# Tile 0 of a fused two-layer kernel: side-by-side remainders, an early gelu table, later weight chunks, and filler matmuls during the convolution

## What is computed

```python
def _attn_ref(x, weight):                      # x (2, 4096, 192), weight (8, 7)
    w = np.exp(weight - np.max(weight, axis=-1, keepdims=True))
    w = w / (np.sum(w, axis=-1, keepdims=True) + 1e-09)
    x_pad = np.concatenate([np.zeros((B, 6, D)), x], axis=1)
    idx = np.arange(S)[:, None] + np.arange(7)[None, :]
    x_unf = x_pad[:, idx, :].reshape(B, S, 7, 8, 24)
    return np.einsum('hk,bskhg->bshg', w, x_unf).reshape(B, S, D)

def _moe_ref(x, w_in, w_out):                  # w_in (192, 2048), w_out (2048, 192)
    h = x @ w_in
    g = h * (1.0 / (1.0 + np.exp(-1.702 * h)))
    return g @ w_out

def _moe2_ref(x, w_in, w_out, a, b):
    h = x @ w_in
    P = a[0] + a[1] * h + a[2] * h**2 + a[3] * h**3
    Q = 1.0 + np.abs(b[0]) * np.abs(h) + np.abs(b[1]) * h**2
    return (P / (Q + 1e-6)) @ w_out

return _moe2_ref(_moe_ref(_attn_ref(x, weight), ...), ...)
```

## Time and profile before

| | us |
|---|---|
| median of 3 runs | 1370.47 |
| lowest and highest | 1369.91, 1372.64 |
| the profiled execution | 1370.77 |
| its span, first to last instruction | 1368.5 |
| PE busy | 1321.6 |
| DVE busy | 1110.2 |
| ACT busy | 966.7 |
| POOL busy | 322.6 |

### The profile page before, as it was taken

The page is one execution under the profiler, slowest core; times in us unless marked ns, Lnnn a source line. Parts: engine busy times, 40 slices in busy tenths (PEclk is TensorE's granted clock), DMA queues, the critical chain, the costliest instruction groups (busy, mean ns, idle before and its releaser), DMA issues. The chain is left out here.

```text
span 1368.5 us, 14943 instructions
## 1 busy us (share of the span) xinstructions
PE 1321.6 (97%) x4800; PEld 698.8 (51%) x4800; DVE 1110.2 (81%) x1223; ACT 966.7 (71%) x1144; POOL 322.6 (24%) x148
## 2 busy tenths in 40 slices
PE   3999999999999999999999999999999999999885
PEld 2445555555555555555555555555555555555431
DVE  4339898888889888888888888888888888877894
ACT  4337777777777777777777777777777777777683
POOL 3202222222222222222222222222222222222222
PEclk9999999999999999999999999999999999999997
DMA  7100000000000000000000000000000000000000
GB/s 198 52 12 0 12 1 24 1 23 1 12 11 0 23 0 23 0 11 11 0 23 0 23 0 11 11 0 23 0 22 3 12 1 0 12 1 12 0 12 11
DMA packets 32884, 20.38 MB, mean 15 GB/s; under 512 B 10321, under 2 KB 30801, under 8 KB 32849
## 3 DMA queue, kind: packets, MB, share of 16 engines
q1 hardware_dynamic: 32372, 19.93, 5.2%
q10 hardware_dynamic: 477, 0.01, 0.0%
HBM read 13.64 MB, written 6.29 MB: 15 GB/s over the span
## 5 line engine op out<-in xcount | busy, mean ns | idle before, releaser
L729 POOL TENSOR_TENSOR work<-work 128x1024 f32<-128x1024 f32 x128 | 303.4, 2370 | 987.8 <-ACT work L470 936.9
L281 PE MATMUL acc_a<-g,down 128*128 128x512 f32 x1024 | 478.5, 608 | 0.0
L281 PEld LDWEIGHTS acc_a<-g,down 128*128 128x128 f32 x1024 | 183.9, 190 | 293.9 <-issue 293.9
L287 PE MATMUL acc_b<-g,down 128*64 128x512 f32 x1024 | 271.6, 607 | 13.9 <-DVE g L630 12.2
L619 DVE TENSOR_TENSOR work<-work,h 128x1024 f32<-128x1024 f32 x128 | 156.4, 1222 | 136.6 <-ACT work L470 135.8
L457 ACT ACTIVATE work<-h,par 128x1024 f32<-128x1024 f32 x128 | 142.7, 1115 | 171.7 <-PE h L275 170.7
L267 PE MATMUL h<-x_a_hi,up_a_hi 128*128 128x512 f32 x512 | 235.0, 459 | 22.3 <-DVE x_b L601 15.5
L497 ACT ACTIVATE work<-work 128x1024 f32<-128x1024 f32 x128 | 135.9, 1062 | 157.3 <-POOL work L729 156.9
L268 PE MATMUL h<-x_a_lo,up_a_hi 128*128 128x512 f32 x512 | 201.8, 394 | 0.0
L269 PE MATMUL h<-x_a_hi,up_a_lo 128*128 128x512 f32 x512 | 201.3, 393 | 0.0
L270 PE MATMUL h<-x_b,up_b_hi 128*128 128x512 f32 x512 | 200.4, 392 | 0.0
(11 more groups left out here) (80 smaller groups left out, 939.2 us busy)
## 6 DMA issues: line engine op xcount, KB each, us to landing
out<-y_out SPq DMA_DIRECT2D x16, 384.0 KB, 2.5
x_in_a<-in_x SPq DMA_DIRECT2D x16, 256.0 KB, 2.8
down<-in_moe_w_out SPq DMA_DIRECT2D x8, 384.0 KB, 6.6
x_in_b<-in_x SPq DMA_DIRECT2D x32, 64.0 KB, 2.5
work<-in_moe_w_in SPq DMA_DIRECT2D x8, 256.0 KB, 4.3
work<-in_moe_w_in SPq DMA_DIRECT2D x16, 128.0 KB, 4.7
wts<-in_weight ACTq DMA_DIRECT2D x2, 0.4 KB
wts<-in_weight SPq DMA_DIRECT2D x2, 1.3 KB
```

The costliest lines, as they stand in the source:

```text
L281: last = mm(l.acc_a[:], l.down[:, f, 0:P], l.g[:, slot, k, :], start=f == 0, stop=f == STEPS - 1)
L287: return mm(acc_b[l.acc_row:l.acc_row + DB, :], l.down[:, f, P:D], l.g[:, slot, k, :], start=f == 0, stop=f == STEPS - 1)
L729: tt(m, sq[(s - LAG_RATIO) % 2], seed, ALU.mult).then_inc(m_ready, 1)
```

## The change

There are four edits, all for the first tile; the loop over the other tiles is as before.

1. In tile 0 (`v1 < DUOS`), `down_b_apart` takes the place of `down_b` for layer 1: unit k = 0 sums on partitions 64 to 127, unit k = 1 on partitions 0 to 63. So each half holds a sum over 8 units, and DVE adds the halves in step n = 8, with a copy and an addition into a new buffer `x2_part`, before it splits.
2. ACT fetches gelu's table in set-up, by a gelu of one column right behind the Sqrt.
3. ACT takes layer 1's weight chunks 2 and 3 behind the gelus of steps 0 and 1 rather than around the split of x. Layer 2's chunks follow in steps 2, 3, 4 and 5.
4. PE runs three fp32 matmuls of 128x512 (the identity with `xt_a`) into `acc_a` once 13 of the convolution's operations are done. Nobody reads their result.

```diff
-S_WEIGHTS2 = (0, 2, 4, 5)
+S_WEIGHTS2 = (2, 3, 4, 5)
+WARM_AFTER = 13
...
+            def down_b_apart(l, d, slot, k):
+
+                row = l.acc_row if k == 0 else DB - l.acc_row
+                return mm(acc_b[row:row + DB, :], l.down[:, 2 * d + k, P:D], l.g[:, slot, k, :],
+                          start=d == 0, stop=d == DUOS - 1)
...
-                        last_b = down_b(L1, e1, (s - LAG_DOWN1) % 2, k)
+                        unit = down_b_apart if isinstance(v1, int) and v1 < DUOS else down_b
+                        last_b = unit(L1, e1, (s - LAG_DOWN1) % 2, k)
...
             pe.wait_ge(x_evacuated, 2)
+            pe.wait_ge(conv_steps, WARM_AFTER)
+            for _ in range(3):
+                mm(L1.acc_a[:], ident[:], xt_a[:, HALO:], start=True, stop=True)
...
             fn(root[:, 1:2], root[:, 0:1], ACT.Sqrt).then_inc(setup_act, 1)
+            act.wait_ge(setup_act, 3)
+            fn(stat[:, 0:1], root[:, 1:2], ACT.Gelu_apprx_sigmoid)
             weights_hi(L1, 1, stage1, w1_hi)
-            weights_hi(L1, 2, stage1, w1_hi)
             split_x1(0, 0)
-            weights_hi(L1, 3, stage1, w1_hi)
...
                     step(i, s, i % 2)
+                    if i == 0 and s < 2:
+                        weights_hi(L1, 2 + s, stage1, w1_hi)
                     if i == 0 and s in S_WEIGHTS2:
                         weights_hi(L2, S_WEIGHTS2.index(s), stage2, w2_hi)
...
                 if s == S_X2 and tile_live(t):
                     dve.wait_ge(acc1_b_done, t + 1)
                     wait(dve, h2_ready, DUOS * (t - 1))
-                    nc.vector.tensor_copy(L2.x_b[DB:P, 1 - p, :], acc_b[DB:P, :]).then_inc(x2_b_hi_done, 1)
+                    whole = acc_b
+                    if isinstance(t, int) and t == 0:
+                        whole = x2_part
+                        nc.vector.tensor_copy(x2_part[DB:P, :], acc_b[0:DB, :]).then_inc(x2_part_read, 1)
+                        dve.wait_ge(x2_part_read, 1)
+                        tt(x2_part[DB:P, :], acc_b[DB:P, :], x2_part[DB:P, :], ALU.add).then_inc(x2_part_added, 1)
+                        dve.wait_ge(x2_part_added, 1)
+                    nc.vector.tensor_copy(L2.x_b[DB:P, 1 - p, :], whole[DB:P, :]).then_inc(x2_b_hi_done, 1)
                     dve.wait_ge(x2_b_hi_done, t + 1)
-                    tt(L2.x_b[0:DB, 1 - p, :], acc_b[DB:P, :], L2.x_b[DB:P, 1 - p, :].bitcast(F32), ALU.subtract)\
+                    tt(L2.x_b[0:DB, 1 - p, :], whole[DB:P, :], L2.x_b[DB:P, 1 - p, :].bitcast(F32), ALU.subtract)\
                         .then_inc(x2_lo_done, 1)
```

More of the change, by code:

```diff
@@ L142, in build_program @@
         y_b = sb("y_b", [P, HALF])
+        x2_part = sb("x2_part", [P, NT])
         y_out = sb("y_out", [P, BLOCKS, D])
@@ L159, in build_program @@
         h1_ready = sem("h1_ready"); g1_ready = sem("g1_ready"); g1_used = sem("g1_used")
+        x2_part_read = sem("x2_part_read"); x2_part_added = sem("x2_part_added")
         acc1_b_done = sem("acc1_b_done"); x2_b_hi_done = sem("x2_b_hi_done")
```

## The result

Over six runs each, the changed kernel took 1361.36 us (median; 1360.97 to 1365.07) and the kernel before 1370.19 (1368.02 to 1372.78). The ratio is 0.9936, 95% interval 0.9923 to 0.995: 8.8 us faster. The profiled execution took 1360.97, its span is 1358.7, against 1368.5 before: 9.8 us less.

What follows compares the result with a forecast made beforehand. The prediction took PE, busy 97% of the span, to set the pace; terms of 2.2, 1.7 and 6.9 us summed to 10.7 unrounded, giving 1359.8 us from the median of 1370.47, range 1358.2 to 1363.2.

Steps and rivals of the forecast that it cites:

- Rival A: Step 0 on PE: the clock is low there despite the filler; gain 9.0 us, time 1361.4; chance 0.30.
- C: Prologue: PE's earlier start does not come, something else ending last; gain 8.5 us, time 1362; chance 0.04.
- Term 1: Prologue: with weight chunks 2 and 3 moved, PE starts at 19.4 instead of 21.56; 2.2 us.
- Term 2: Step 0: the filler raises PE's clock, so the step takes 2.81 us instead of 4.50; 1.7 us, 0 as other end.
- Term 3: Tile 0, n = 1 to 8: paired 64-column units on different halves save 0.86 us a step; 6.9 us.
- Sum at n = 9: PE's first step that is the same as before: it stands 10.7 us earlier, down_b at 70.7 instead of 81.41.
- The table: ACT's set-up: the early gelu table load costs 0; without it ACT would lose 2 us at the first gelu.
- What has to stay hidden: Tiles 0 and 1: DVE's added halves (some 1.4 us in hand), POOL's low parts and tile 1's convolution; cost 0.
- The step that failed: Whole span: PE sets the pace, so time gained in prologue or tile 0 arrives undiminished at the end.
- a difference at the end that is smaller than at n=9: Kernel's end against step n=9: named as a sign that the prediction is wrong; no size given.

Runs made afterwards that it cites:

- e5: The changed kernel without the three filler matmuls on PE; 1365.06 us, ratio 0.9957 to the kernel before.
- e1: The changed kernel run again unaltered, as yardstick; 1362.65 us, ratio 0.9944 to the kernel before.
- e4: The changed kernel with 60 one-column memsets added on DVE in the set-up (336 instructions ahead of its loop); 1359.90 us, ratio 0.993 to the kernel before.
- e8: The changed kernel without the set-up's gelu that loads the table early; 1363.92 us, ratio 0.9935 to the kernel before.
- e3: The kernel before with two one-column memsets added on DVE in the set-up; 1372.73 us against 1370.92, ratio 1.0009.
- e7: The changed kernel with ACT's weight chunks where they were before, filler and early table kept; 1367.90 us, ratio 0.9975 to the kernel before.
- e11: The changed kernel with ACT's weight chunks where they were before and without the filler; 1366.65 us, ratio 0.996 to the kernel before.
- e6: The changed kernel with tile 0's remainders one behind the other as before, without the two additional DVE operations; 1365.84 us, ratio 0.9954 to the kernel before.
- e2: The changed kernel with two DVE instructions fewer ahead of the loop (274, not 276); 1360.02 us, ratio 0.993 to the kernel before.

## Why the prediction was right, and where it was not

The measured 1361.36 lies within the range of 1358.2 to 1363.2, and 1.6 us above the 1359.8. The terms of the head were right, each by its own mechanism. That the sum held at the end is in part luck: the range was wide because of rivals A and C, which did not come, and this width took in a loss of 2.4 us that no rival named. Two of the six runs, 1364.27 and 1365.07, lie above it.

- **Term 1, PE's start (2.2):** PE started at 19.37, forecast 19.4; 2.19 less than 21.56. Right for this pair of executions, and by the way forecast: convolution, DVE's weights, three subtractions. Probably too large as an average, since the start in the old order was 20.3 to 21.6 in four executions.
- **Term 2, the clock (1.7):** the first gelu is at 22.12, forecast 22.2. Measured by itself 1.59 (e5). The filler ran at the low clock for nearly all its 5.29 us, and the gap behind it was 0.78. In e1 it took 4.26 and left 1.82 us, and step 0 still ran high. Rival A, which had 0.30, did not come about in any of the eight profiled executions with the filler and the new chunk order, but it was close: in e4 and e8 the filler took 5.46 us, low to its end, and the trace's record of the clock, which begins with its first change, begins at 19.15 and 18.80, 0.2 and 0.6 us ahead of step 0. What was missing is that step 1 can be low too in the old order (e3, e7, e11), so that the filler and the early start save more in some executions.
- **Term 3, the pairs (6.9):** 6.80 (e6).
- **Sum at n = 9 (10.7):** 10.75.
- **The table:** the text said that without it ACT would lose 2 us. Wrong: that took the old place of the load, behind chunk 3, over into an order in which chunk 3 has left. In the new order ACT is idle from 18.2 to 22.1 and the load fits (e8: 0 us).
- **What has to stay hidden:** x_b's low part ended at 68.26 + 0.69 = 68.95, 1.7 us ahead of `down_b` at 70.66. No new wait for POOL or ACT came up: the three of 1.6 us for gelu are those of the earlier trace rows.
- **The step that failed** is the first one: that whatever is gained in the head "arrives undiminished at the end, as long as no other engine is late for it". I had asked which engine would be late in tiles 0 and 1 and priced edit 1's two DVE instructions by their time there (cost 0). Their price was their place in the program: four fetches that PE waits 0.6 us for each, 2.4 us in the middle (e2, e3 and e4 show it). The prediction had named this as a sign of being wrong, "a difference at the end that is smaller than at n=9", and it came about: 9.8 against 10.75. The rest of the difference to the forecast is the tail, in which the clock gave 1.5 us in the profiled execution and takes it back in others.

## What to carry to other kernels

An engine's instructions ahead of a loop can have a price even when they fill idle time: here two on DVE made the middle 2.9 us longer (e3), and 60 beyond them made it 2.6 us shorter again (e4 against e1). Compare the packet count of the instruction queue between two versions, and look at the first operation of the body in the second pass; if it is late and a wait of much the same length repeats with the loop's period, take an instruction out or put some in. Put a filler for the clock close to the work: it held over gaps of 0.6 to 1.8 us in eight executions and not over 3.39 us in one. It is read in the durations of the matmuls that follow it.

## What the runs showed of the hardware

**DVE's loop is fetched again in its passes or not, by the count of instructions ahead of it.** 274 or 336 DVE instructions ahead of a body of 299: 16 packets on q14 and none of its cost; 276: 36 packets of 8 KB, 3.5 to 3.8 us from the branch to the body's first instruction instead of 0.3, and 0.6 to 0.9 us of waiting on PE in four of five passes. The releaser that the views name for L634 is PE, which had been done for 0.8 us.

**The clock at PE's start and in the tail differs between executions of the same kernel.** The changed kernel's profiled execution in the last tile:

```profile
1347.70 1.93 PE L290 MATMUL acc_b<-g,down 128*64 128x512 f32 x4 [3.49 <-DVE g L652]
1349.56 1.98 PE L284 MATMUL acc_a<-g,down 128*128 128x512 f32 x4
1353.12 0.41 PE L316 MATMUL turned<-ident,y_a 128*128 128x128 f32 x2 [1.58 <-ACT y_a L524]
```

and e1, the same kernel:

```profile
1348.79 3.67 PE L290 MATMUL acc_b<-g,down 128*64 128x512 f32 x4 [3.49 <-DVE g L652]
1352.39 2.88 PE L284 MATMUL acc_a<-g,down 128*128 128x512 f32 x4
1356.85 0.41 PE L316 MATMUL turned<-ident,y_a 128*128 128x128 f32 x2 [1.58 <-ACT y_a L524]
```

After the same idle 3.49 us, four records took 1.93 us in the one, at a granted clock of 1.00 (1347.5 to 1349.5), and 3.67 in the other, at 0.50 (1349.5 to 1351.5), which makes 5.42 or 8.06 us to the first transposition; the tails of all profiled executions lie between 88.2 and 92.6 us. In these two they are 88.6 and 92.6: 2.6 us of the 4.0 arise at this place, the rest earlier and later in the tail. The tail thus accounts for the two spans of one kernel, 1358.7 and 1362.8, and it is why a gain of 1 or 2 us is better read from the parts of the span than from five runs.
